# An attention and two-MLP kernel: bias and scale of each exponential from one two-column VectorE operation, and q scaled by 1/8 on GpSimd

## The reference

```python
scale = 1.0 / np.sqrt(D)                       # D = 64, so 1/8
q_bucket, k_bucket = hash of the signs of q @ proj, k @ proj      # 6 bits
mask = q_bucket[:, :, :, None] == k_bucket[:, :, None, :]
scores = scale * np.matmul(q, k.transpose(0, 1, 3, 2))
scores = np.where(mask, scores, -1000000000.0)
scores = scores - np.max(scores, axis=-1, keepdims=True)
attn = np.exp(scores)
attn = attn / (np.sum(attn, axis=-1, keepdims=True) + 1e-09)
x = np.matmul(attn, v)                         # 2 batches, 8 heads, 768 rows, D = 64
x = ((x @ w1) * (x @ w2) @ w3) @ w_out         # first MLP
out = (sigmoid(x @ w_gate) * (x @ w_val)) @ moe2_w_out
```

## Time and profile before

| what | value |
|---|---|
| time, median of 3 runs | 761.7 us (758.96 to 762.28) |
| the profiled execution's own time | 763.15 us |
| its span, first to last instruction | 761.4 us |
| granted TensorE clock, mean | 0.996 of full speed |
| busy: PE, DVE, ACT, POOL | 735.6, 466.0, 465.4, 358.0 us |

### The profile page before, as it was taken

The page is one execution under the profiler, slowest core; times in us unless marked ns, Lnnn a source line. Parts: engine busy times, 40 slices in busy tenths (PEclk is TensorE's granted clock), DMA queues, the critical chain, the costliest instruction groups (busy, mean ns, idle before and its releaser), DMA issues.

```text
span 761.4 us, 12753 instructions
## 1 busy us (share of the span) xinstructions
PE 735.6 (97%) x4136; PEld 674.0 (89%) x4136; DVE 466.0 (61%) x1015; ACT 465.4 (61%) x857; POOL 358.0 (47%) x299
## 2 busy tenths in 40 slices
PE   6799999999999998899999999999999999999998
PEld 4588888889787787899999999999999999988886
DVE  5789999999999898544144635532333335764000
ACT  5789999999998987633537225645345354705100
POOL 3867374653739599444646400235635644240000
PEclk9899999999999999999999999999999999999999
DMA  5682644527273300110010000001100010501001
GB/s 148 222 186 62 164 106 116 151 70 195 82 182 77 91 29 0 50 35 29 31 51 28 1 1 1 26 31 29 51 32 28 31 52 0 166 1 69 28 28 41
DMA packets 26609, 51.80 MB, mean 68 GB/s; under 512 B 4160, under 2 KB 12688, under 8 KB 26576
## 3 DMA queue, kind: packets, MB, share of 16 engines
q1 hardware_dynamic: 26272, 51.32, 24.7%
q10 hardware_dynamic: 304, 0.07, 0.0%
HBM read 29.43 MB, written 3.15 MB: 43 GB/s over the span
## 4 chain that ended last, share of the span: by engine, by line
PE 72%; DVE 10%; issue 6%; ACT 5%; SPq 2%; DMA 2%; POOL 1%; DVEq 0%; ACTq 0%; POOLq 0%
PE pair_bank L1328 14%; PE pair_bank L1330 14%; PE pair_bank L1329 14%; PE bank L1330 6%; PE bank L1329 6%; PE bank L1328 6%; PE bank L1241 4%; PE pair_bank L1229 4%; PE bank L1256 3%; DVE rowmax L943 3%; DVE pt_lo L976 3%; ACT prob L670 2%; DMA sq<-q_codes 1%; ACT pt_hi L630 1%; PE bank L1290 1%
## 5 line engine op out<-in xcount | busy, mean ns | idle before, releaser
L1094 DVE TENSOR_TENSOR u<-bank,u 128x384 f32<-128x384 f32 x80 | 44.4, 556 | 136.5 <-ACT u L630 126.8
L630 ACT ACTIVATE u<-pair_bank 128x384 f32<-128x384 f32 x120 | 58.6, 491 | 106.9 <-PE pair_bank L1330 106.8
L976 DVE TENSOR_TENSOR pt_lo<-bank,pt_hi 128x384 fp32r<-128x384 f32 x192 | 97.5, 549 | 6.6 <-ACT pt_hi L630 6.3
L670 ACT ACTIVATE prob<-pair_bank,ebias,escale 128x768 f32<-128x768 f32 x96 | 95.3, 992 | 6.0 <-DVE ebias L954 6.0
L1229 PE MATMUL pair_bank<-mk,sq 128*128 128x384 f32 x384 | 92.3, 363 | 6.1 <-ACT prob L670 1.9
L630 ACT ACTIVATE pt_hi<-bank 128x384 fp32r<-128x384 f32 x192 | 85.0, 491 | 18.0 <-PE bank L1241 15.5
L943 DVE TENSOR_REDUCE rowmax<-pair_bank 128x1 f32<-128x768 f32 x96 | 91.0, 948 | 5.1 <-PE pair_bank L1229 5.1
L1241 PEld LDWEIGHTS bank<-ident,prob 128*128 128x128 f32 x576 | 65.2, 141 | 28.8 <-DVE pt_lo L976 13.1
L1241 PE MATMUL bank<-ident,prob 128*128 128x128 f32 x576 | 84.4, 280 | 6.5 <-ACT prob L713 2.8
L1328 PE MATMUL pair_bank<-y_hi,g_hi 128*128 128x384 f32 x240 | 80.3, 335 | 0.0
L1229 PEld LDWEIGHTS pair_bank<-mk,sq 128*128 128x128 f32 x384 | 62.8, 191 | 16.4 <-issue 10.3
(11 more groups left out here) (165 smaller groups left out, 1976.5 us busy)
## 6 DMA issues: line engine op xcount, KB each, us to landing
sq<-hl SPq DMA_DIRECT2D x45, 192.0 KB
mk<-hl SPq DMA_DIRECT2D x15, 384.0 KB
qk_raw<-in_qk SPq DMA_DIRECT2D x7, 768.0 KB, 5.5
w_raw<-in_w SPq DMA_DIRECT2D x16, 256.0 KB, 2.7
v_raw<-in_v SPq DMA_DIRECT2D x16, 192.0 KB, 2.7
wo_raw<-in_wo SPq DMA_DIRECT2D x12, 256.0 KB, 3.7
out<-out_sb SPq DMA_DIRECT2D x12, 256.0 KB, 2.0
mk<-hl SPq DMA_DIRECT2D x15, 192.0 KB
```

The lines of the kernel that those rows point to most:

```text
L630: return act.activation(dst, src, ACT.Copy)
L670: act.activation(prob[k % 3][:, :].rearrange("p (c n) -> p c n", c=KC), pair_bank[k % 2][:, :, 0:HALF], ACT.Exp, bias=ebias[:, k:k + 1], s ...
L976: dve.tensor_tensor(pt_lo[(k // UQ) % 2][cut], t_bank[j][:, 0:384].rearrange("p (t n) -> p t n", t=3), pt_hi[(k // UQ) % 2][cut].bitcast(F ...
```

## The change

The scale of 1/8 is put into q before the scores are made, so the exponential's scale becomes 1 or 0. `row_max` writes minus the maximum into column 0 of `neg_max[:, k, :]`, whose column 1 holds a constant 1. One scalar_tensor_tensor, `exp_inputs`, compares column 0 with 2^29 and multiplies the result with both columns: `exp_in[:, k, 0]` is the bias and `exp_in[:, k, 1]` the scale. It stands where `exp_scale` stood; `exp_bias` is gone. Its two tensor inputs, `neg_max[:, k, 0:1]` broadcast to two columns and `neg_max[:, k, :]`, both lie in SBUF.

In `qk_split` GpSimd treats k first, then waits for `bits_done`, scales q in place by two more 128x384 tensor_tensor operations, and goes on with q. For pair 0 ScalarE's two copies of 128x768 become four of 128x384, and VectorE's one subtraction over 128x1536 becomes two over 128x768. The diff, blank lines left out:

```diff
@@ -105,12 +105,13 @@
         shift = at("shift", [128, 1], F32, CONST + 1408)
         zeros = at("zeros", [128, 1, 1], F32, CONST + 1440)
         penalty = at("penalty", [128, 1], F32, CONST + 1472)
-        rowmax = at("rowmax", [128, STEPS], F32, CONST + 1024)
-        escale = at("escale", [128, STEPS], F32, CONST + 1088)
-        ebias = at("ebias", [128, STEPS], F32, CONST + 1152)
+
+        neg_max = at("neg_max", [128, STEPS, 2], F32, CONST + 1024)
+        exp_in = at("exp_in", [128, STEPS, 2], F32, CONST + 1120)
         rowsum = at("rowsum", [128, STEPS], F32, CONST + 1216)
         rowsum_eps = at("rowsum_eps", [128, STEPS], F32, CONST + 1280)
         rnorm = at("rnorm", [128, STEPS], F32, CONST + 1344)
+        scale = at("scale", [128, 1, 1], F32, CONST + 1504)
         wo1_raw = at("wo1_raw", [128, KF, DM], F32, WP)
         wp = at("wp", [128, KF, DM], F32, WP)
         wp_lo = at("wp_lo", [128, KF, DM], F32R, WP)
@@ -221,6 +222,7 @@
             return ctx.enter_context(nc.semaphore(name))
         first_parts, qk_first = sem("first_parts"), sem("qk_first")
+        ones_set = sem("ones_set")
         zeroed, consts_ready, proj_loaded = sem("zeroed"), sem("consts_ready"), sem("proj_loaded")
         shift_loaded = sem("shift_loaded")
         qk_loaded, qk_hi_done, hl_ready = sem("qk_loaded"), sem("qk_hi_done"), sem("hl_ready")
@@ -229,7 +231,8 @@
         v_loaded = [sem("v_loaded_a"), sem("v_loaded_b")]
         v_hi_done = [sem("v_hi_done_a"), sem("v_hi_done_b")]
         v_ready = [sem("v_ready_a"), sem("v_ready_b")]
-        s_done, max_done, escale_done, ebias_done = sem("s_done"), sem("max_done"), sem("escale_done"), sem("ebias_done")
+        s_done, max_done, exp_in_done = sem("s_done"), sem("max_done"), sem("exp_in_done")
+        q_scaled = sem("q_scaled")
         exp_done, eps_done, rnorm_done = sem("exp_done"), sem("eps_done"), sem("rnorm_done")
         norm_done = [sem(f"norm_done{j}") for j in range(UQ)]
         t_done, pt_hi_done, pt_lo_done = sem("t_done"), sem("pt_hi_done"), sem("pt_lo_done")
@@ -447,8 +450,16 @@
                     pool.wait_ge(first_parts, 10)
                 at_least(pool, assembled[0], copied(0, p - 1))
                 pool.wait_ge(assembled[1], copied(1, p - 1))
-                pieces = [(t, slice(HALF * hf, HALF * hf + HALF)) for t in range(2) for hf in range(2)]
-                for t, cols in pieces:
+                pieces = [(t, slice(HALF * hf, HALF * hf + HALF)) for t in (1, 0) for hf in range(2)]
+                for n, (t, cols) in enumerate(pieces):
+                    if n == 2:
+                        pool.wait_ge(bits_done, p + 1)
+                        for _, half in pieces[2:]:
+                            pool.tensor_tensor(one(qk_raw[:, 0, half]), one(qk_raw[:, 0, half]),
+                                               scale[:, :, :].broadcast_to([128, 1, HALF]),
+                                               ALU.mult).then_inc(q_scaled, 1)
+                    if t == 0:
+                        pool.wait_ge(q_scaled, 2 * p - 3 + n)
                     rounded(one(hl[:, 2 * t, cols]), one(qk_raw[:, t, cols])).then_inc(qk_hi_done, 1)
                 for n, (t, cols) in enumerate(pieces):
                     pool.wait_ge(qk_hi_done, 4 * p - 2 + n)
@@ -584,8 +595,9 @@
             pool.memset(ident[:, :], 0.0).then_inc(zeroed, 1)
             pool.memset(zeros[:, :, :], 0.0).then_inc(zeroed, 1)
+            pool.memset(scale[:, :, :], SCALE).then_inc(zeroed, 1)
             pool.memset(penalty[:, :], PEN).then_inc(zeroed, 1)
-            pool.wait_ge(zeroed, 3)
+            pool.wait_ge(zeroed, 4)
             pool.affine_select(out=ident[:, :], in_=ident[:, :], compare_op=ALU.not_equal, fill=1.0, base=0,
                                pattern=[[-1, 128]], channel_multiplier=1).then_inc(consts_ready, 1)
             pool.wait_ge(consts_ready, 1)
@@ -628,6 +640,9 @@
         def _(act):
             def copy(dst, src):
                 return act.activation(dst, src, ACT.Copy)
+
+            def scaled(dst, src):
+                return act.activation(dst, src, ACT.Copy, scale=SCALE)
             def pair_raw_high(unit, j):
@@ -665,11 +680,11 @@
             def exp(p, k):
                 s = STEPS * p + k
-                act.wait_ge(ebias_done, s + 1)
+                act.wait_ge(exp_in_done, s + 1)
                 at_least(act, t_done, 2 * (s - 2))
                 act.activation(prob[k % 3][:, :].rearrange("p (c n) -> p c n", c=KC),
-                               pair_bank[k % 2][:, :, 0:HALF], ACT.Exp, bias=ebias[:, k:k + 1],
-                               scale=escale[:, k:k + 1], accum_out=rowsum[:, k:k + 1]).then_inc(exp_done, 1)
+                               pair_bank[k % 2][:, :, 0:HALF], ACT.Exp, bias=exp_in[:, k, 0:1],
+                               scale=exp_in[:, k, 1:2], accum_out=rowsum[:, k:k + 1]).then_inc(exp_done, 1)
             def transposed_hi(p, k):
                 s = STEPS * p + k
@@ -733,13 +748,15 @@
             for hf in range(2):
                 act.dma_start(shift[64 * hf:64 * hf + 64, :], shift_d[:, :]).then_inc(shift_loaded, 16)
             act.wait_ge(qk_first, 16)
-            copy(hl[:, 0::2, 0:HALF], qk_raw[:, :, 0:HALF])
+            copy(hl[:, 2, 0:HALF], qk_raw[:, 1, 0:HALF])
+            scaled(hl[:, 0, 0:HALF], qk_raw[:, 0, 0:HALF])
             act.wait_ge(qk_loaded, 16)
-            copy(hl[:, 0::2, HALF:SEQ], qk_raw[:, :, HALF:SEQ]).then_inc(qk_hi_done, 1)
+            copy(hl[:, 2, HALF:SEQ], qk_raw[:, 1, HALF:SEQ])
+            scaled(hl[:, 0, HALF:SEQ], qk_raw[:, 0, HALF:SEQ]).then_inc(qk_hi_done, 1)
             copy(mk[0][D:2 * D, 0, :], qk_raw[0:D, 1, :]).then_inc(first_parts, 1)
-            copy(sq[0][0:D, 0, :], qk_raw[0:D, 0, :]).then_inc(first_parts, 1)
-            copy(sq[0][0:D, 1, :], qk_raw[0:D, 0, :]).then_inc(first_parts, 1)
+            scaled(sq[0][0:D, 0, :], qk_raw[0:D, 0, :]).then_inc(first_parts, 1)
+            scaled(sq[0][0:D, 1, :], qk_raw[0:D, 0, :]).then_inc(first_parts, 1)
             act.wait_ge(rows_set[0], 2)
             act.wait_ge(codes_done, 1)
             for hf in range(2):
@@ -940,19 +957,14 @@
             def row_max(p, k):
                 s = STEPS * p + k
                 dve.wait_ge(s_done, s + 1)
-                dve.tensor_reduce(rowmax[:, k:k + 1], pair_bank[k % 2][:, :, 0:HALF], AX.XY,
-                                  ALU.max).then_inc(max_done, 1)
-
-            def exp_scale(p, k):
+                dve.tensor_reduce(neg_max[:, k, 0:1], pair_bank[k % 2][:, :, 0:HALF], AX.XY, ALU.max,
+                                  negate=True).then_inc(max_done, 1)
+
+            def exp_inputs(p, k):
                 dve.wait_ge(max_done, STEPS * p + k + 1)
-                dve.tensor_scalar(escale[:, k:k + 1], rowmax[:, k:k + 1], -PEN / 2, SCALE, ALU.is_gt,
-                                  ALU.mult).then_inc(escale_done, 1)
-
-            def exp_bias(p, k):
-                dve.wait_ge(escale_done, STEPS * p + k + 1)
-                dve.tensor_scalar(ebias[:, k:k + 1], rowmax[:, k:k + 1], escale[:, k:k + 1], -1.0, ALU.mult,
-                                  ALU.mult).then_inc(ebias_done, 1)
+                dve.scalar_tensor_tensor(exp_in[:, k, :], neg_max[:, k, 0:1].broadcast_to([128, 2]),
+                                         PEN / 2, neg_max[:, k, :], ALU.is_lt, ALU.mult).then_inc(exp_in_done, 1)
             def sum_eps(p, k):
                 dve.wait_ge(exp_done, STEPS * p + k + 1)
@@ -1032,10 +1044,8 @@
                         row_max(*nxt)
                     sum_eps(p, k)
                     if nxt:
-                        exp_scale(*nxt)
+                        exp_inputs(*nxt)
                     inverse(p, k)
-                    if nxt:
-                        exp_bias(*nxt)
                     if k not in NORM_ON_ACT:
                         normalise(p, k)
                     if k > 0:
@@ -1048,12 +1058,15 @@
                         x_operand_low(T3, 0)
                         x_operand_low(T3, 1)
+            dve.memset(neg_max[:, :, 1:2], 1.0).then_inc(ones_set, 1)
             code_rows(dve, 0)
+            dve.wait_ge(ones_set, 1)
             dve.wait_ge(shift_loaded, 32)
             code(0)
             dve.wait_ge(qk_hi_done, 1)
-            dve.tensor_tensor(hl[:, 1::2, :], qk_raw[:, :, :], hl[:, 0::2, :].bitcast(F32),
-                              ALU.subtract).then_inc(hl_ready, 1)
+            dve.tensor_tensor(hl[:, 3, :], qk_raw[:, 1, :], hl[:, 2, :].bitcast(F32), ALU.subtract)
+            dve.scalar_tensor_tensor(hl[:, 1, :], qk_raw[:, 0, :], SCALE, hl[:, 0, :].bitcast(F32), ALU.mult,
+                                     ALU.subtract).then_inc(hl_ready, 1)
             dve.wait_ge(rows_set[0], 2)
             dve.wait_ge(codes_done, 1)
@@ -1065,8 +1078,7 @@
             dve.tensor_copy(sq[0][D:2 * D, 0, :], hl[0:D, 1, :].bitcast(F32)).then_inc(first_parts, 1)
```

(3 more changed lines are left out.)

## The result

The changed kernel takes 784.17 us (median of 4 runs, 782.43 to 787.71) against 761.7: a ratio of 1.0302, 95% interval 1.0264 to 1.0340. It is slower by 22.5 us; the forecast was 20.4 slower, 782.1. The profiled execution took 782.43 us with a span of 780.6. The direction and the mechanism held. The terms of the sum held less well.

A forecast was written before the change was run, and what follows sets the result against it. VectorE was taken to bound the stretch beside GpSimd's list, with PE and ScalarE nearly full. 761.7 + (0.9+1.7+0.3+0.8+5x2.1+3.2+4.0-1.0 = 20.4) = 782.1 us, range 766 to 800.

The forecast's parts named there:

- The operation that decides: exp_inputs on VectorE, two SBUF inputs: waits until GpSimd's current instruction is over, whatever its size; 0.5 us taken each.
- Rivals 1 and 2: First: so small an operation is exempt, 760.6 us, chance 0.10; second: whole saving every step, no wait, 754.5 us, 0.03.
- rival 3: GpSimd's next instruction gets in first, so each wait is near 0.9 us: 799 us, chance 0.09.
- The steady pair: Five waits of 0.5 us beside GpSimd's list less 0.4 saved: 2.1 us more per pair; later waits counted as hidden.
- The signs of the forecast for this pair: Profile of a steady pair: 35.5 us instead of 33.4, VectorE busy all through, PE idle 2 us.
- The saving of 0.4: VectorE's bound stretch per pair without exp_bias: three steps save 0.12 us, four with normalise 0.01.
- The last pairs: From 234.4 us to attention's end: 3.2 us more, then 4.0 in the last pair (7.2 less 3.2 hidden by PE).
- Pair 0 and the start: Start's cut subtraction 0.9 us, pair 0's later copies 1.7, GpSimd held up 0.3, two waits from 49.6 to 67.4 0.8.
- The tail: Behind attention: some GpSimd work is out of VectorE's way, 1.0 us gained.
- rival 4: Copies of assemble(0) come late and take over; with the small operation exempt from waiting 766 us, chance 0.03.

The follow-up runs named there:

- e3: Changed kernel with the new operation's first tensor input a constant in PSUM, so only one input in SBUF: 768.0 us, ratio 1.0096.
- e4: Kernel before with exp_scale's factor 1/8 read from an SBUF column as a second tensor input, nothing else changed: 782.63 us, ratio 1.0272.
- e6: e5 without GpSimd's two scalings of q (q of pairs 1 to 7 unscaled): 759.55 us, ratio 0.9978.
- e9: Kernel before without the addition of 1e-9 to the row sum, one small VectorE operation fewer per step: 757.66 us, ratio 0.9947.
- e10: Changed kernel with the new operation placed behind the inverse instead of ahead of it: 790.84 us, ratio 1.0401.
- e5: e3 with GpSimd's subtraction for v of pair 0 waiting for both halves of VectorE's subtraction at the start: 767.47 us, ratio 1.0097.
- e2: Kernel before with q scaled on GpSimd and the cut start as in the changed kernel, both small operations kept: 767.06 us, ratio 1.0081.
- e1: Changed kernel without GpSimd's two scalings of q and their wait (q of pairs 1 to 7 unscaled): 783.81 us, ratio 1.0307.

## Why the prediction was right, and where its sum was not

**The operation that decides: right.** The wait doesn't shrink with the size of the operation. Minimum 0.149, maximum 1.83 and a sum of 43.7 us lie where the forecast put them (near 0.15, above 0.9, 35 to 60). e3 takes the second SBUF input away and the wait is gone; e4 adds one to the kernel before and the loss is there. Rivals 1 and 2 fall with these rows, rival 3 with the mean of 0.455. The rule of the Trainium skill that the prediction weighed (SBUF — State Buffer, "Who interferes with whom") held for operations of one and two columns. The same section says that issue order and not shape decides who blocks. The row at 74.84 agrees as to shape, with 1.83 us for an operation of 0.15. As to order it agrees for the first GpSimd instruction alone: the second starts at 75.60, 0.76 us behind the operation's own start, and still goes first.

**The steady pair: over-sized.** I had 5 x 0.5 - 0.4 = 2.1 us; a pair lost 1.2 in four of five cases, 2.0 in the first, so 6.8 for 10.5. The step that failed is the price of a wait taken as that of any moment. GpSimd's list has the forecast length, 16.3 us (168.06 to 184.37), and five of the new operations fall into it. One steady pair of the changed kernel, these five and the sixth behind the list, then the first two normalises:

```profile
170.32 0.16 DVE L966 SCALAR_TENSOR_TENSOR exp_in<-neg_max 128x2 f32<-128x2 f32 x1
...
172.93 0.29 DVE L966 SCALAR_TENSOR_TENSOR exp_in<-neg_max 128x2 f32<-128x2 f32 x1
...
175.34 0.23 DVE L966 SCALAR_TENSOR_TENSOR exp_in<-neg_max 128x2 f32<-128x2 f32 x1
...
178.73 0.86 DVE L966 SCALAR_TENSOR_TENSOR exp_in<-neg_max 128x2 f32<-128x2 f32 x1
...
181.71 0.64 DVE L966 SCALAR_TENSOR_TENSOR exp_in<-neg_max 128x2 f32<-128x2 f32 x1
...
188.05 0.96 DVE L966 SCALAR_TENSOR_TENSOR exp_in<-neg_max 128x2 f32<-128x2 f32 x1
```

```profile
175.69 1.07 DVE L980 TENSOR_SCALAR prob<-prob,rnorm 128x768 f32<-128x768 f32 x1
...
182.46 1.04 DVE L980 TENSOR_SCALAR prob<-prob,rnorm 128x768 f32<-128x768 f32 x1
```

The five hold 0.01, 0.14, 0.08, 0.71 and 0.49 us of wait, 1.43 and not 2.5. An operation that has waited comes out at the end of a GpSimd instruction, and with steps of constant length the next ones meet GpSimd at a fixed phase and not at any moment: in the four steady pairs from 102.23 on each of these lengths repeats within 0.02 us. And a second effect that I hadn't counted: the two normalises took 1.49 and 1.46 us before and take 1.07 and 1.04 now, 0.84 us less. Part of the new wait is the old one, moved. 1.43 - 0.84 - 0.4 is only 0.2, though, and the pair lost 1.2. The sixth operation, beside the second `w3_split`, held 0.81 us more, and the prediction had counted those there as hidden. With it the sum is 1.0, or 0.8 with the saving of 0.56 that e6 measured; the rest of the 1.2 isn't accounted for. That the sixth isn't hidden is argued from this sum, not shown by a run of its own; what the trace shows is that VectorE now idles 1.40 us in the pair, against 0.37, so that waits in some steps are not made good in others. The signs of the forecast for this pair were off in the same way: 34.60 us and not 35.5, VectorE not busy all through it, and PE idle for 0.9 us and not for 2.

**The saving of 0.4: a little small, and its meaning wrong.** I worked it out from distances between starts. Measured without waits it is 0.56 (e6), and for another small operation 0.4 (e9). The distances had two misreadings. Without `exp_bias` the inverse of the changed kernel starts 0.07 to 0.08 us ahead of the large operation (103.96 and 104.04) and not 0.13, so a step without normalise saves 0.17. And the 0.19 us between 103.95 and 104.14 aren't those of a bare pair: `exp_scale` starts between them, at 104.07. In e10, where nothing stands between the two, it is 0.17 (104.81 and 104.98); the saving of 0.01 in a step with normalise holds all the same, as its inverse and normalise start 0.19 apart in most steps of the changed kernel. By these distances the sum is 3 x 0.17 + 4 x 0.01 = 0.55. In e6 and e9 the pair is then nearly filled by PE (32.54 of 32.84, 32.60 of 32.99), and both also shed waits of normalise. The room that PE left before, 33.40 - 33.05 = 0.35, would have told that little could come of any saving on VectorE; that 0.56 came goes with PE's busy time, which fell to 32.54.

**The last pairs: under-sized.** From the last mark to the MLPs I had 3.2 + 4.0 = 7.2; it was 9.9. One instruction of GpSimd, then three of VectorE, of which the last is a normalise that is held too; and the stretch by engine, in e3 and in before:

```profile
288.71 1.85 POOL L520 TENSOR_TENSOR g_raw_lo<-g_raw,g_hi 128x768 fp32r<-128x768 f32 x1
...
288.82 1.77 DVE L966 SCALAR_TENSOR_TENSOR exp_in<-neg_max 128x2 f32<-128x2 f32 x1
290.51 0.15 DVE L976 RECIPROCAL rnorm<-rowsum_eps 128x1 f32<-128x1 f32 x1
...
293.54 2.10 DVE L980 TENSOR_SCALAR prob<-prob,rnorm 128x768 f32<-128x768 f32 x1
```

```profile
232.27:298.34 66.07, 60.72 (x345) 50.33 (x345) 60.42 (x138) 59.84 (x118) 59.80 (x48) 1.00 0.23 54
```

```profile
230.26:294.85 64.59, 60.20 (x346) 50.31 (x346) 59.97 (x158) 59.89 (x118) 56.42 (x45) 1.00 0.23 55
```

GpSimd's instruction started 0.11 us before the operation, so that nearly the whole of it was waited for, 1.62 us, and not half. In the last pair seven operations wait (1.29, 1.45, 1.57, 1.77, 0.73, 1.29 and 1.24 us long): they are held 1.18 us on average, 8.3 in all, where I had 8 x 0.9 = 7.2. The eight ahead of them are held 3.4, where I had 7 x 0.5 = 3.5. Together that is 11.7 for 10.7. In e3, where these waits are gone, the stretch takes 66.1 us instead of 74.5, so of the 11.7 us they cost 8.4, and about the 3.2 that I let vanish did vanish (e3's own operation is 0.07 us longer, which can hide up to 1.3 more). The larger part of the miss is a term that I put at nothing: e3 without the waits still takes 1.5 us more than before, where the sum had a saving of 0.3. The scaling is in it, as e5 takes 65.9 us there and e6, which is e5 without it, 64.3.

**Pair 0 and the start: the sum right, its terms not shown.** 0.9 + 1.7 + 0.3 + 0.8 = 3.7 us were expected up to the third mark, and 3.6 came. The rows of the start are as foreseen. GpSimd's instruction gets in between the halves of the subtraction, and SyncE's first copy is issued at 11.31 instead of 10.32:

```profile
8.61 1.00 DVE L1067 TENSOR_TENSOR hl<-qk_raw,hl 128x768 fp32r<-128x768 f32 x1
8.86 1.60 POOL L474 TENSOR_TENSOR v_st<-v_raw,v_st 128x384 fp32r<-128x384 f32 x1
9.53 1.76 DVE L1068 SCALAR_TENSOR_TENSOR hl<-qk_raw,hl 128x768 fp32r<-128x768 f32 x1
...
11.31 1.82 SPq L343 DMA_DIRECT2D sq<-hl  x3
```

But the terms don't stand by themselves. The scaling with the cut start moved the third mark by 6.2 us in e2, while the scaling taken out in e1 gave 1.8 back (66.89 to 65.08); and e1 and e5 show that what is gained in pair 0 is given back in the steady pairs. The scores of pair 1 start at 51.88 in the changed kernel, not near 52.5, and PE waits for no copy there. So the copies of rival 4 weren't late in the changed kernel; in e2 they were, in pair 0 alone, where PE waited 5.3 us for them.

**The tail: right.** Behind attention 1.1 us are gained, where -1.0 was expected. The addition of the earlier trace rows, 2.20 us beside GpSimd, now runs free of it, as its line shows; that this makes the 1.1 us is argued, not tested:

```profile
L994 DVE TENSOR_TENSOR x_f<-x_f,x_tmp x2: 543/544/546, 321.7 to 324.5; 128x384 f32<-128x384 f32 x1, 64x384 f32<-64x384 f32 x1
```

So 3.6 + 6.8 + 9.9 - 1.1 is 19.2, the difference of the two spans, and the match with 20.4 rests on errors that offset each other: 3.7 too much in the steady pairs, 2.7 too little in the last stretch. The closeness of the total is luck to that extent; the mechanism is not.

## What to carry to other kernels

Before a small VectorE operation gets a second tensor input, look where its inputs lie: with both in SBUF it waited here for GpSimd's tensor_tensor instructions, and the price is GpSimd's instruction, not its own (16 us by e3 and 21 by e4 for 96 operations of 0.15 us). One input in PSUM (e3, never over 0.221 us), or a scalar operand in the place of a tensor (`exp_bias`, never over 0.217), avoids it. Price such waits by the durations of the other engine's list in each stretch and expect phase, not an average; and before a saving is counted, read how much room the next-fullest engine leaves. A step that could be dropped, the 1e-9, gained 3.3 us here (e9); the two that were merged cost 22.5, and 6.6 with the waits taken out (e3).

## What the runs showed that I had not expected

- An operation can wait through two GpSimd instructions: 1.83 us beside 0.82 and 1.01, where it came 0.03 us after the first began. It didn't get in at the seam between them. At 288.82 it waited through one of 1.85 and came next; which of the two happens when is left open.
- The pair has discrete lengths. In e3 and e5 it takes 33.2 to 33.3 or 33.9 to 34.0 us with the same instructions, by whether one normalise waits 0.85 or 1.62 us; a gain of 1.3 us upstream vanished into that in e5.
- GpSimd's scaling costs 7.9 us where the small operations don't wait (e5 against e6) and 0.4, within noise of nothing, where they do (the changed kernel against e1). Two parts of a change that were measured alone, 5.6 us in e2 and 22.4 in e1, don't add up to the whole, 22.5.
- Twelve small operations fewer in a pair shift the phase of the large ones against GpSimd: the normalise of step 6 takes 1.46 us before and 0.61 in e9, for an edit that doesn't touch it.
